# At the border between two expert layers: three waits moved in a fused mLSTM and MoE kernel

## What is computed

```python
def _moe_ref(x, w_gate, w_noise, noise, w1, w2):
    noisy_logits = x @ w_gate + np.log1p(np.exp(x @ w_noise)) * noise
    top2 = np.argpartition(-noisy_logits, 2, axis=1)[:, :2]
    ...
    for e in range(E):
        for k in range(2):
            mask = top2[:, k] == e
            h = np.maximum(x[mask] @ w1[e], 0.0)
            out[mask] += top2_w[mask, k, None] * (h @ w2[e])

def _moe2_ref(x, domain_probs, w1, w2):
    p = domain_probs / (domain_probs.sum(-1, keepdims=True) + 1e-09)
    for e in range(E):
        h = np.maximum(x @ w1[e], 0.0)
        out += p[:, e:e + 1] * (h @ w2[e])
```

## Time and profile before

| | us |
|---|---|
| median of 3 runs | 702.77 |
| lowest and highest | 700.76 and 704.07 |
| the profiled execution, its time | 704.07 |
| the profiled execution, its span in the trace | 701.9 |
| PE busy in the span | 684.1 (97%) |
| PE's weight loads busy | 625.6 (89%) |
| DVE busy | 390.4 (56%) |
| ACT busy | 288.9 (41%) |
| POOL busy | 106.1 (15%) |

### The profile page before, as it was taken

One profiled execution on the slowest core, in us unless ns is written; L12 is line 12 of the kernel. 1 busy time (PEld: TensorE's weight loads), 2 busy tenths in 40 slices (PEclk: granted clock), 3 DMA queues, 4 the chain that ended last, 5 costly groups with the idle time before them and its releaser, 6 DMA issues.

```text
span 701.9 us, 11335 instructions
## 1 busy us (share of the span) xinstructions
PE 684.1 (97%) x4297; PEld 625.6 (89%) x4297; DVE 390.4 (56%) x656; ACT 288.9 (41%) x494; POOL 106.1 (15%) x145
## 2 busy tenths in 40 slices
PE   9999998999999999999899999999999999999997
PEld 7888885999999999999788988998889898999986
DVE  6677765666665654653655455545545545454422
ACT  5544624554444544543443333423324332342311
POOL 7433202522021020014202002012000001000000
PEclk9999999999999999999999999999999999999999
DMA  7446761755644647921563424435234152331001
GB/s 227 117 114 168 207 188 38 197 180 151 195 130 127 190 165 266 346 86 56 183 188 106 135 75 127 127 107 157 76 106 126 54 149 99 105 117 48 0 0 38
DMA packets 28810, 92.52 MB, mean 132 GB/s; under 512 B 4672, under 2 KB 10816, under 8 KB 28768
## 3 DMA queue, kind: packets, MB, share of 16 engines
q1 hardware_dynamic: 21472, 76.22, 36.3%
q0 software_dynamic: 3072, 10.49, 5.2%
q10 hardware_dynamic: 4224, 5.24, 2.1%
HBM read 76.87 MB, written 15.07 MB: 131 GB/s over the span
## 4 chain that ended last, share of the span: by engine, by line
PE 90%; DVE 3%; DMA 2%; ACT 2%; issue 1%; SPq 1%; POOL 0%; DVEq 0%; POOLq 0%; ACTq 0%
PE pY L1351 13%; PE pY L1353 13%; PE pY L1352 12%; PE pH L1336 10%; PE pH L1337 10%; PE pH L1338 10%; PE pH L1343 5%; PE pH L1341 5%; PE psYa L1223 2%; PE psD L1138 2%; DMA stage<-in_w 1%; PE pT L1313 1%; PE psL L1266 1%; PE psS L1158 1%; PE psYa L1243 1%
## 5 line engine op out<-in xcount | busy, mean ns | idle before, releaser
L648 ACT ACTIVATE h_hi<-pH 128x512 fp32r<-128x512 f32 x160 | 96.0, 600 | 276.1 <-PE pH L1343 272.1
L1018 DVE SCALAR_TENSOR_TENSOR h_lo<-pH,h_hi 128x512 fp32r<-128x512 f32 x160 | 110.6, 691 | 163.8 <-ACT h_hi L648 157.7
L1351 PE MATMUL pY<-w_hi,h_hi 128*128 128x320 f32 x608 | 189.0, 311 | 2.0 <-DVE h_lo L1018 0.7
L1353 PE MATMUL pY<-w_hi,h_lo 128*128 128x320 f32 x608 | 187.5, 308 | 0.0
L1352 PE MATMUL pY<-w_lo,h_hi 128*128 128x320 f32 x608 | 187.5, 308 | 0.0
L1336 PE MATMUL pH<-x_hi,w_hi 128*128 128x512 f32 (+3 forms) x324 | 122.9, 379 | 1.2 <-issue 1.2
L788 DVE TENSOR_TENSOR w_lo<-stage,w_hi 128x1024 fp32r<-128x1024 f32 (+1 forms) x80 | 108.6, 1358 | 26.6 <-ACT w_hi L575 26.4
L1351 PEld LDWEIGHTS pY<-w_hi,h_hi 128*128 128x128 f32 x608 | 114.1, 188 | 10.2 <-issue 5.6
L1337 PE MATMUL pH<-x_lo,w_hi 128*128 128x512 f32 (+3 forms) x324 | 120.3, 371 | 0.0
L1338 PE MATMUL pH<-x_hi,w_lo 128*128 128x512 f32 (+3 forms) x324 | 120.0, 370 | 0.0
L1352 PEld LDWEIGHTS pY<-w_lo,h_hi 128*128 128x128 f32 x608 | 114.1, 188 | 3.3
(11 more groups left out here) (265 smaller groups left out, 652.5 us busy)
## 6 DMA issues: line engine op xcount, KB each, us to landing
stage<-in_w SPq DMA_DIRECT2D x40, 640.0 KB, 4.3
stage<-in_w SPq DMA_DIRECT2D x40, 512.0 KB, 3.5
stage<-in_w SPq DMA_DIRECT2D x40, 256.0 KB
results_by_slot<-X SPq DMA_DIRECT2D x9, 640.0 KB, 9.1
results_by_slot<-acc ACTq DMA_DIRECT2D x8, 640.0 KB, 3.2
qk<-in_qk_t SPq DMA_DIRECT2D x16, 240.0 KB
kv<-in_kv_n SPq DMA_DIRECT2D x8, 480.0 KB
og<-in_o_n SPq DMA_DIRECT2D x2, 960.0 KB, 6.6
```

The lines of the kernel that those rows point to most:

```text
L648: act.activation(HH[s % 2][:, :], pH[s % 2][:, :], ACT.Relu).then_inc(hh_done[layer], 1)
L1018: dve.scalar_tensor_tensor(out=HL[s % 2][:, :], in0=pH[s % 2][:, :], scalar=0.0, in1=f32(HH[s % 2][:, :]), op0=ALU.max, op1=ALU.subtract). ...
L1351: pe.matmul(y[:, 0:XD], hh, wh, start=(f == 0), stop=False)
L1353: return pe.matmul(y[:, 0:XD], hl, wh, start=False, stop=(f == NF - 1))
```

## The change

Three waits change place; no operation on data is added or removed.

```diff
@@ SP
-            sp.wait_ge(layer1_mm, 1)
+            sp.wait_ge(gathered[1][1], 32)
             for u in range(1, E2):
                 load_second(u, u)
@@ DVE
             dve.sem_inc(hl_done[1], H_CREDIT)
+            dve.wait_ge(layer1_mm, 1)
             for tt in range(BT):
                 near_1, near_2 = (t[:, tt % 2, :] for t in near_G[tt // 2])
                 dve.wait_ge(last_out, tt + 1)
...
-            dve.wait_ge(layer1_mm, 1)
             for half in range(2):
@@ PE
-            pe.wait_ge(rt_tiles, 2)
-            used = pe.value_load(counts[0:1, 0:1], min_val=MUST, max_val=V1)
             pe.wait_ge(sel_made, ST)
             for tt in range(BT):
...
                 ins.then_inc(last_mm, 1)
+            pe.wait_ge(rt_tiles, 2)
+            used = pe.value_load(counts[0:1, 0:1], min_val=MUST, max_val=V1)
             with pe.If(used > MUST):
```

## The result

The changed kernel takes 710.15 us in the median of 3 runs (709.64 to 713.24), before 702.77: a ratio of 1.0121, 95% interval 1.0086 to 1.0156. It is slower by 7.4 us by the medians and by 8.5 us by the ratio, which here rests on three executions of each kernel. The forecast said slower by 3.8 and put 0.57 on slower than 0.5%; the sign was right, the size about half, and the time lies outside the range that was given (704.6 to 709.0). One of the rivals, the fetch that drowns in the loads, had 0.12 and describes what happened to the branch: it grew by 2.7 us, within the 2 to 4 named there.

What follows compares the result with a forecast made beforehand. The prediction took PE's branch over the conditional block to bound the border between the expert layers. Its terms, 0.6 + 0.5 + 2.5 + 0.2 = 3.8 us, gave 706.6 us against the median of 702.77, range 704.6 to 709.0.

Steps and rivals of the forecast that it cites:

- What bounds the border: Between the expert layers, PE's 4143 ns branch over the conditional block holds its first turning matmul, not DVE's mix.
- A, the register load: On PE, moved between the last selection matmul and the branch, the load has no cover and adds 0.6 us.
- B, the early loads: SP's second-expert loads start at 335.4 instead of 341.28, gain nothing, and their traffic lengthens PE's branch by 0.5 us.
- these three parts: PE's branch read as 1.0 us until its instruction fetch begins, 1.7 us of fetch, 1.3 us until the program goes on.
- Rival 2: At PE's branch, the fetch drowns in the loads: branch up to twice as long, 5 to 7 us slower in all; chance 0.12.
- C, the mixes behind the signal: DVE's eight mixes wait for PE's `layer1_mm`, so the second half's turning and first `up` come 2.5 us later.
- D, the clock: At the border PE stands still longer, so its low-clock stretch may reach the first `up` matmuls: 0.2 us.
- The sum and its base: Border terms 0.6 + 0.5 + 2.5 + 0.2 = 3.8 us: profiled 704.07 becomes 707.9, or 706.6 against the median 702.77.
- Layer 2: From its first `up` to the end, unchanged; a different length would mean an effect the forecast lacks.
- the first (nothing reaches the branch): Load and traffic don't reach PE's branch; only the later mixes cost, 2.0 to 2.7 us, 705.2; chance 0.20.
- the fourth (a short branch): PE's branch was a single long one; at 0.2 us, `up` starts 1.1 us earlier, 701.6; chance 0.05.
- The third (the clock stays low into the first visit): PE's clock stays low into layer 2's first visit: 3.6 + 1.5 = 5 us slower, 707.9; chance 0.14.

Runs made afterwards that it cites:

- no_block: The kernel before without PE's conditional block of spare visits, so no branch or fetch at the border; ratio to the kernel before 1.0010 (0.9982 to 1.0038).
- dve_pe: The changed kernel with SP's edit undone, so the second expert's loads wait for `layer1_mm` again; ratio to the kernel before 1.0069 (1.0048 to 1.0089).
- pe_only: The kernel before with only PE's register load moved between the last selection matmul and the branch; ratio 1.0042 (1.0020 to 1.0064).
- pe_mid_store: The kernel before with PE's register load moved ahead of the branch and ACT's last store started behind the third scaling, not the second; ratio 1.0008 (0.9981 to 1.0035).
- sp_only: The kernel before with only SP's edit: the second expert's loads wait for the gathers instead of `layer1_mm`; ratio 1.0054 (1.0031 to 1.0077).
- dve_only: The kernel before with only DVE's wait for `layer1_mm` moved ahead of the eight mixes; ratio 1.0034 (1.0013 to 1.0056).

## Why the prediction was right or wrong

- **What bounds the border**: right, and shown by no_block. The branch held PE; the releaser named by the profile was a coincidence of 0.04 us. What I did not have was the next in line, ACT's register load, nor ACT's wait for the store. Removing the branch gained nothing measurable, though no_block lets the loads start early as well.
- **A, the register load**: 0.6 us was said, and 0.6 is what it put ahead of the branch. The step that failed was to take its effect as a mere shift. With the branch 0.6 us later, the fetch no longer slipped in before the store but came behind it, and the branch grew by 1.0 us (dve_pe, pe_only; undone in pe_mid_store). That microsecond is counted in the next item. A delay of a request can cost more than the delay.
- **B, the early loads**: this is the step with most of the error. I said +0.5 us, with an upper bound of +1.7, and it was 2.7 (of which 1.0 would have come by the store alone). I priced the fetch's own packet, as if its time would be shared between streams. The packet got shorter, 0.93 us instead of 1.73; what grew was the wait before it, from 1.0 to 4.5 us. I had even split the branch in these three parts, and varied only the middle one. Rival 2 had the right size (2 to 4 us) and too little chance, on the argument that the fetch of before already shared with the store. It had hardly shared: its packet started just ahead of the store's (6 packets in that tenth of a microsecond). That the loads would gain nothing was right.
- **C, the mixes behind the signal**: 2.5 said, 2.1 measured. The spacing alternates between 0.59 and 0.47 us when nothing is waited for (the rows above), and I had used the first of them, read from a pair, for all seven.
- **D, the clock**: 0.2 said, 0.7 measured in the profiled execution. The turning was as slow as before, as said. But the low stretch lasted 10.2 us and ran 1.5 us into the first `up`s.
- **The sum and its base**: 0.6 + 2.7 + 2.1 + 0.7 = 6.1 us at the border, while the medians differ by 7.4. I applied the profile's difference to the median of before. The profiled execution of before was itself 1.3 us above that median, and had a fall of the clock in it that 28 of 96 executions don't have. None of the changed kernel's 15 executions lies in that group. That is my reading of the remaining 1.3; it is not measured apart, and the spread of a median of three is as large. So that part of the miss stays open.
- **Layer 2** from its first 512-column matmul to the end: unchanged, 350.42 and 350.45, as said. (PE is busy for 45.0 of the 45 us from 355 to 400; the 35.0 given for that stretch belongs to 35 us.)

Of the rivals, the first (nothing reaches the branch) is excluded by sp_only and dve_pe, the fourth (a short branch) by every profile that has the branch: 3.3 to 7.0 us, never short. The third (the clock stays low into the first visit) came true beside the second, with 0.7 us instead of 1.5.

The Trainium skill's "Runtime: NRT & Kernel Launch", section on instruction fetch mechanics, says that a taken branch out of the loaded window has to fetch its target first; no_block agrees, where branch and packet are gone together.

The measured wait for the fetch's packet was 2.7 us behind the store and 3.7 to 4.5 us beside the loads, against 0.9 with a clear way. So the store adds 1.8 us and the loads add 2.8 to 3.6. The Trainium skill's "DMA: Bandwidth & Descriptors", section on queues, rings and completion order, says that a DMA engine goes round its queues packet by packet, and that a packet is typically 9 to 17 descriptors. What the profile counts as a packet is smaller: those of the store hold 1.3 KB, one row of 320 values, so I take each for one descriptor, which no run shows. They took 0.055 us each (265 in 91.6% of 16 us), those of the loads 0.22 us (81 in 109.9% of 16 us, sp_only). As an estimate with that page's 9 to 17, one turn of the store is 0.5 to 0.9 us and one of the loads 2.0 to 3.7 us. Beside the loads one such turn is about what was measured. Behind the store the measured 1.8 us are two turns or more, and there the measurement decides.

## What to carry to other kernels

In this kernel, a jump over a long block of code was a DMA transfer in disguise, and stood on the engine's path. Where you find such a jump, look at the branch's own duration in the sequencer's rows, find its packet on the instruction queue, and ask of every transfer that a change moves whether it now runs in front of that packet. Keep a wait that looks too strict when what it holds back is bulk traffic without a deadline; here `layer1_mm` on SP kept 2.9 MB out of the way of a 16 KB fetch and of a store that another engine waits for. And put a wait no earlier in an in-order engine's program than the first operation that needs it: eight mixes went from hidden to exposed by one moved line.

## What the runs showed of the hardware

- The branch over some 400 rows of PE's program took 3.3 us with nothing in the way: 0.9 us until the fetch packet started, 0.93 us for the packet, 1.4 to 1.5 us until the program went on. Beside the early loads it took 6.3 to 7.0 us.
- The wait of 0.9 us is with idle DMA engines; behind a store of 640 KB it was 2.7 us (dve_pe, pe_only), once 1.4 us in the middle of that store (dve_only), and beside 2.9 MB of loads 3.7 to 4.5 us. The packet's own duration varied only from 0.93 to 1.73 us.
- A TENSOR_LOAD of one register took 313 to 323 ns on PE where it reads `counts`, 484 to 493 where it reads `code`, and on ACT 479 to 482 in nine profiles and 1026 to 1724 in five.
- A pause of PE of 0.6 us was followed by a fall of the clock 2 to 3 us later in some executions of the same kernel and not in others, and cost 3 us in 32 matmuls and more behind them. In four profiles the clock also fell near 19 us; in pe_mid_store PE had been busy there for 16.52 of 16.60 us.
- One of SP's four output DMA starts took 1.3 to 1.8 us in five of the 14 profiles instead of at most 0.44, and the span was about 1 us longer.
